# A schedule of eight-step slots for the attention groups, and other steps and layouts for the weight pieces, in a fused attention and two-layer MLP kernel

## Chip, cores and metric

One core of one Trainium2 chip runs the whole program. The metric is the device time of one execution in microseconds, the median of several.

## What is computed

Inputs: q, k, v of 8 batches x 8 heads x 576 tokens x 64, phi of 8 x 8 x 576 x 32, and four weight matrices.

```python
a = softmax(phi)                    # over the 32 memory slots of a token
k_m, v_m = a^T k, a^T v             # per head, 32 x 64
attn = softmax(q k_m^T / 8)         # 576 x 32
x = attn v_m                        # tokens x 512, 4608 tokens
h1 = x @ w1_in                      # 512 -> 2048
x1 = where(h1 > 0, h1, exp(min(h1, 0)) - 1) @ w1_out        # 2048 -> 512
h2 = x1 @ w2_in
out = (h2 * clip(h2 + 3, 0, 6) / 6) @ w2_out
```

Everything is float32.

## The kernel before

Every large product is made of three matmul passes over two fp32r parts of each operand (a "hi" part, which ScalarE casts, and a "lo" part, the rest): `three_passes`, lines 435 to 437, on PE. The program has four large passes, one after the other on PE: *up 1*, *down 1*, *up 2*, *down 2*. Between them the hidden values go to DRAM and come back.

**Up 1 with the attention (`batch`, 8 batches of 16 steps).** A step is one column block of the hidden layer: PE makes 12 matmuls of 128x288 (`up1`), ACT makes two activations (lines 771 and 773), DVE one operation (line 1053, `g_made`), SP stores the result (`store_h`). PE begins a step only when the g of two steps before is made. The product v_m x w1_in is not taken per token; it is folded into the weights: an *item* (8 per batch) is two plain matmuls on PE (line 524), a cast on ACT (763, hi part) and a difference on DVE (1044, lo part, `w1_lo_made`), and the next item waits for the lo part of the one before. The attention goes in groups of four heads, two groups per batch, 16 in all. Groups 0 and 1 are made in the *opening*, ahead of the first step. The others are made between the steps, cut into twelve stages: on the side of the values S_PHI (row maxima, DVE), S_MAX, S_SUB (DVE difference, ACT exponential), S_SUM (POOL), S_KV (24 matmuls, then two DVE operations for the inverse and copies on ACT and DVE), S_KMT (two transposes, copies of kmT and vT on ACT); on the side of the queries S_Q0, S_Q1 (six transposes each, copies on ACT and DVE), S_SC (24 matmuls, then two DVE operations), S_EXP (ACT), S_NORM (DVE, then `normalise` on POOL), S_PT (six transposes, then pT_hi on ACT and pT_lo on DVE).

What sets the order is a table written out by hand, `FIRST_BATCH` for batch 0 and `BATCH` for the others: at step f of batch b, `stages_at(b, f)` names the stages of the groups 2b+2 (EVEN), 2b+3 (ODD) and 2b+4 (NEXT); `items_at(b, f)` names the item. All five engines walk the same lists in the same order after their part of the step, each on its own instruction queue. In `BATCH`, S_SC stands at steps 4 and 10, S_PT at 9 and 15; items stand at steps 0, 2, 3 and, for the next batch, 5, 9, 11, 13 and 14. Step 0 of a batch waits for pT_lo of its own second group, which was made at step 15. The transposed scores and queries share two PSUM banks, so S_Q0 waits until pT_lo of the group before is made (EVEN) or other operations of it (ODD).

POOL also prepares *pieces* (`make_piece`): forms of w1_out and of a part of w2_out, seven sums of 128x128 blocks each in hi and lo, for a scheme with seven products in place of eight. SP loads the three blocks (`load_piece`), POOL makes sums, cast and difference, SP stores the piece to DRAM (`store_piece`). `PIECE_LOADS`, `PIECE_SUMS`, `PIECE_STORES` give their steps. Two pieces make a *tile* (1792 KB), eight tiles make a matrix. In DRAM a tile has 14336 contiguous bytes per partition, so `load_tile` moves 128 runs of 14336 bytes; a piece store moves runs of 7168 bytes.

**Down 1 (`y_block`, 9 blocks of 14 grains)** keeps the eight tiles of w1_out in SBUF; the pieces of w2_in go through `stage_b` meanwhile. In the last block ACT requests tiles 0 to 3 of w2_in one after the other (line 791, `load_tile(1, j)`), and tiles 4 to 7 after its casts for up 2. SP stores the last `y_sb` (layer 1's output), then waits for that store before it requests the input of batch 1 (`load_xc(1, 1)`) and goes on.

**Up 2 (`up_block`, 8 batches u of 8 steps f)**: a step is seven products of six matmuls 128x288. ACT copies one of them into `c_sum` (line 860, `up_first`), makes the gates (867) and the first activation into `eg` (876, `up_c11`); DVE makes the sums (1201 to 1226) and, at f == 2, the four sums of the next batch's input (`xc_sums`, 1184 to 1189); SP stores `eg` (`store_g`, line 1602). There are two `eg` buffers, and `up_c11` of step n waits until the store of step n-2 has landed. `c_sum` 1 and 2 and both `eg` share SBUF with `y_sb` or `stage_b`, so `up_first` of step 1 waits for the last store of `y_sb`. In batches 1 to 6 two pieces of w2_out are made per batch through the single `stage_c`: SP requests them ahead of steps 0 and 3 (`out_piece`, which first waits until the piece before it is stored), ACT casts at f == 2 and 7 (778), POOL makes sums and lo, SP stores at f == 2 and f == 7. SP's own queue is in order: `out_piece` at f == 0 stands ahead of `store_g(u, 0)`. In the last batch SP first requests three inputs of down 2 of 1 MB each (line 1627), then stores `eg`; ACT requests one tile of w2_out after each step (`load_tile(2, f - 1)`).

**Down 2 (`down_block`, 9 blocks of 14 grains)** uses these tiles; its second grain waits for tiles 4 to 7.

## Time and profile before

| what | us |
|---|---|
| median of 3 runs | 1719.53 |
| the runs | 1712.4 to 1724.2 |
| profiled execution, its time | 1714.28 |
| its span | 1712.6 |
| opening | 0 to 48 |
| up 1 with the attention | 48 to 518 |
| down 1 | 518 to 884 |
| up 2 | 884 to 1330 |
| down 2 | 1330 to 1712 |

The rows further down come from the profiled execution. Times in them count from the start of its span; 1.7 us of its time lie around the span. PE is TensorE (PEld its weight loads), DVE VectorE, ACT ScalarE, POOL GpSimd, SPq the queue of SyncE. "L437" is line 437. A bracket at the end of a timeline row is the engine's idle time before it and what ended it. PEclk is the granted TensorE clock as a share of 2.4 GHz.

### The profile page before, as it was taken

How to read it: one execution, taken by the hardware profiler on the slowest of the kernel's cores; microseconds unless marked ns; L12 is line 12 of the kernel's file. 1: busy time of each engine (PE TensorE's matmuls, PEld its weight loads, DVE VectorE, ACT ScalarE, POOL GpSimd, SP SyncE). 2: the span in 40 equal slices, each digit the busy share in tenths (PEclk: the TensorE clock that was granted, in tenths of full speed). 3: DMA queues.
4: the chain of work that ended last, by engine and by line, in shares of the span. 5: the costliest groups of instructions: out<-in, count | busy, mean ns of one | idle time of the engine just before them, and what ended most of it. 6: DMA issues, size and time to landing. Idle time of an engine off the chain costs nothing.

```text
span 1712.6 us, 30373 instructions
## 1 busy us (share of the span) xinstructions
PE 1537.7 (90%) x12080; PEld 1445.6 (84%) x12080; DVE 1098.6 (64%) x1528; ACT 730.2 (43%) x1037; POOL 262.1 (15%) x278
## 2 busy tenths in 40 slices
PE   6888887988979999999986999899987799999999
PEld 4666666766769999999986999899986799999998
DVE  4555555555547788888854666666645577777775
ACT  2555645555654444444422334343332333333333
POOL 0243433334200000000001233433220000000000
PEclk9989989998989999999997999999998899999999
DMA  8466678767576555555556444444468543333331
GB/s 243 145 189 213 208 244 263 222 229 231 198 265 239 194 184 178 197 189 178 172 228 250 150 162 170 147 154 179 160 223 313 192 135 129 122 122 122 122 126 46
DMA packets 193853, 318.26 MB, mean 186 GB/s; under 512 B 9456, under 2 KB 140528, under 8 KB 190704
## 3 DMA queue, kind: packets, MB, share of 16 engines
q1 hardware_dynamic: 189872, 285.81, 50.0%
q10 hardware_dynamic: 3904, 31.43, 5.0%
q8 instruction: 48, 0.79, 0.2%
q14 instruction: 29, 0.24, 0.0%
HBM read 178.78 MB, written 138.41 MB: 185 GB/s over the span
## 4 chain that ended last, share of the span: by engine, by line
PE 67%; DVE 11%; DMA 9%; ACT 6%; issue 4%; SPq 1%; POOL 0%; ACTq 0%; DVEq 0%
PE ps L435 21%; PE ps L437 20%; PE ps L436 20%; DMA layer_hidden<-eg 3%; PE ps L496 2%; DMA forms_out<-forms_c 2%; ACT e L773 2%; PE ps L524 2%; DVE g L1053 2%; ACT e L771 2%; PE ps L458 2%; DMA layer_out<-y_sb 1%; DVE ga_lo L1267 1%; DMA tile<-forms_out 1%; ACT ga_hi L918 1%
## 5 line engine op out<-in xcount | busy, mean ns | idle before, releaser
L435 PE MATMUL ps<-xc_hi,tile 128*128 128x288 f32 x896 | 275.0, 307 | 60.8 <-DVE c_sum L1201 58.5
L435 PE MATMUL ps<-tile,ga_lo 128*128 128x256 f32 x1008 | 288.9, 287 | 14.5 <-DMA tile<-forms_out 9.3
L435 PE MATMUL ps<-ring_hi,tile 128*128 128x256 f32 x1008 | 286.1, 284 | 3.0 <-DMA tile<-forms_out 3.0
L436 PE MATMUL ps<-tile,ga_hi 128*128 128x256 f32 x1008 | 287.0, 285 | 0.0
L437 PE MATMUL ps<-tile,ga_hi 128*128 128x256 f32 x1008 | 286.9, 285 | 0.0
L436 PE MATMUL ps<-ring_lo,tile 128*128 128x256 f32 x1008 | 285.2, 283 | 0.0
L437 PE MATMUL ps<-ring_hi,tile 128*128 128x256 f32 x1008 | 285.2, 283 | 0.0
L436 PE MATMUL ps<-xc_lo,tile 128*128 128x288 f32 x896 | 272.2, 304 | 0.0
L437 PE MATMUL ps<-xc_hi,tile 128*128 128x288 f32 x896 | 271.0, 302 | 0.0
L435 PEld LDWEIGHTS ps<-xc_hi,tile 128*128 128x128 f32 x896 | 175.8, 196 | 63.9 <-DVE c_sum L1201 61.1
L1053 DVE SCALAR_TENSOR_TENSOR g<-e,ps 128x576 f32<-128x576 f32 x128 | 95.7, 749 | 187.6 <-ACT e L773 180.0
L435 PEld LDWEIGHTS ps<-tile,ga_lo 128*128 128x128 f32 x1008 | 195.3, 194 | 17.9 <-issue 12.6
L435 PE MATMUL ps<-pT_hi,w_lo 128*128 128x288 f32 x512 | 168.0, 328 | 39.0 <-issue 18.9
L435 PEld LDWEIGHTS ps<-ring_hi,tile 128*128 128x128 f32 x1008 | 193.4, 192 | 3.5 <-issue 3.1
L436 PEld LDWEIGHTS ps<-tile,ga_hi 128*128 128x128 f32 x1008 | 195.4, 194 | 0.0
L437 PEld LDWEIGHTS ps<-tile,ga_hi 128*128 128x128 f32 x1008 | 195.2, 194 | 0.0
L436 PEld LDWEIGHTS ps<-ring_lo,tile 128*128 128x128 f32 x1008 | 193.5, 192 | 0.0
L437 PEld LDWEIGHTS ps<-ring_hi,tile 128*128 128x128 f32 x1008 | 193.5, 192 | 0.0
L437 PEld LDWEIGHTS ps<-xc_hi,tile 128*128 128x128 f32 x896 | 176.3, 197 | 0.0
L436 PEld LDWEIGHTS ps<-xc_lo,tile 128*128 128x128 f32 x896 | 176.1, 196 | 0.0
L918 ACT CAST ga_hi<-a 128x1024 fp32r<-128x1024 f32 x90 | 94.2, 1049 | 176.8 <-PE ps L437 154.6
L436 PE MATMUL ps<-pT_lo,w_hi 128*128 128x288 f32 x512 | 157.4, 307 | 0.0
(178 smaller groups left out, 2788.0 us busy)
## 6 DMA issues: line engine op xcount, KB each, us to landing
layer_hidden<-g SPq DMA_DIRECT2D x128, 288.0 KB, 2.7
x<-layer_hidden SPq DMA_DIRECT2D x36, 1024.0 KB, 5.1
layer_hidden<-eg SPq DMA_DIRECT2D x64, 576.0 KB, 3.0
a<-layer_hidden SPq DMA_DIRECT2D x36, 1024.0 KB, 7.4
forms_out<-forms_a SPq DMA_DIRECT2D x20, 896.0 KB, 4.5
tile<-forms_out SPq DMA_DIRECT2D x8, 1792.0 KB, 12.7
forms_in<-forms_b SPq DMA_DIRECT2D x16, 896.0 KB, 5.5
tile<-forms_in ACTq DMA_DIRECT2D x8, 1792.0 KB, 21.1
```

What stands on the lines that cost most here:

```text
L435: nc.tensor.matmul(dst, a_lo, b_hi, start=first, stop=False, skip_group_check=onto)
L436: nc.tensor.matmul(dst, a_hi, b_lo, start=False, stop=False, skip_group_check=onto)
L437: return nc.tensor.matmul(dst, a_hi, b_hi, start=False, stop=last, skip_group_check=onto)
L458: nc.tensor.matmul(t.ps_kv[rows], t.rows_a[0:ROWS, h, j], t.kv[0:ROWS, :, h, j], start=(j == 0), stop=(j == CH - 1))
L496: mm = nc.tensor.matmul(t.ps_scores[:, h, 2 * j:2 * j + 2], t.qT[:, h // 2, at:at + ROWS], t.kmT[:, h], start=True, stop=True)
L524: mm = nc.tensor.matmul(ps[lm, bank, 0:BANK], vT[:, gi, lm], w_in_raw[:, 2 * gi + p, cols], start=True, stop=True)
L771: nc.scalar.activation(e1[f % 2][:], ps[:, 2 * (f % 2):2 * (f % 2) + 2, 0:HALF], ACT.Relu, scale=-1.0).then_inc(r_made, 1)
L773: nc.scalar.activation(e1[f % 2][:], e1[f % 2][:], ACT.Exp, scale=-1.0).then_inc(e_made, 1)
L918: nc.scalar.copy(ga_hi[grain_slot(q)][:], grain_source(parity, q)).then_inc(grain_hi_made, 1)
L1053: nc.vector.scalar_tensor_tensor(g1[f % 4][:], e1[f % 2][:], -1.0, ps[:, 2 * (f % 2):2 * (f % 2) + 2, 0:HALF], ALU.add, ALU.max).then_inc( ...
L1267: nc.vector.tensor_tensor(ga_lo[slot][:], grain_source(parity, q), ga_hi[slot][:].bitcast(F32), ALU.subtract).then_inc(grain_ready, 1)
```

## The change

1. **Slots.** The two tables go. From batch 0, step 12 on, groups go in slots of eight steps that run on across batches: in the slot of group g its query stages stand at steps 0, 1, 2, 4, 5, 7 (Q0, Q1, SC, EXP, NORM, PT), and the value stages of group g+1 at 0, 1, 3, 4, 6, 7 (PHI, MAX, SUB, SUM, KV, KMT). With respect to a batch a slot begins at step 4 and at step 12. The first twelve steps of batch 0 are two slots of six. The value stages of group 2 are made in the opening (`EARLY`). Group 15 ends at step 11 of batch 6, before at 15.
2. **Items** at steps 1, 3 (the batch's own last two) and 5, 7, 9, 11, 13, 15 (six of the next batch) in plain order; in batch 0 at 0 to 3 and then the same. Six of a batch's items, not five, are made in the batch before. vT has four buffers, not two.
3. **Waits of PE.** S_Q0 always waits for pT_lo of the group before; the extra waits of S_SC and S_PT go.
4. **Pieces of w1_out**: loads at steps 0, 3, 9, sums at 2, 5, 11, stores at 4, 7, 14 (before 0, 6, 12; 2, 8, 14; 5, 11, 1).
5. **Layout** of the forms in DRAM: [j][s][l][partition][896], so each piece store and tile load moves runs of 3584 bytes (four per partition and tile).
6. **Start of up 2**: ACT requests tiles 0 and 1 in the last block of down 1, tile 2 after its casts, tiles 3 to 7 at steps 0 to 4. `y_sb` and `stage_b` trade places and `c_sum`, `eg` move, so that the last store of `y_sb` is waited for by `up_c11` of step 1 and `up_first` of step 2. SP requests `load_xc(1, 1)` ahead of its wait for that store.
7. **Batches 1 to 6 of up 2**: ACT's second cast and SP's second piece store go from f == 7 to f == 6. POOL's calls are written in another form in the same order.

```diff
-    forms = [nc.dram_tensor(f"forms_{n}", (FH, P, 2, 2 * 7 * P), F32, kind="Internal").ap() for n in ("out1", "in2", "out2")]
+    forms = [nc.dram_tensor(f"forms_{n}", (FH, 2, 2, P, 7 * P), F32, kind="Internal").ap() for n in ("out1", "in2", "out2")]
...
+        vT = place("vT", [4, P], F32, at + 2560)
...
-        at = t0 + 5 * TILE
+        at = tail - 2 * FB * WS - 2 * PT_BYTES
...
-        stage_b = stage("_b", tail + 3 * SUB * 8 + DC * BLOCK * 4)
+        stage_b = stage("_b", tail + 3 * SUB * 8)
...
-        y_sb = place("y_sb", [DC, BLOCK], F32, tail + 3 * SUB * 8)
+        y_sb = place("y_sb", [DC, BLOCK], F32, tail + 3 * SUB * 8 + PIECE)
...
-        c_sum = [place(f"c_sum{i}", [3, HALF], F32, tail + 3 * i * ring1) for i in range(3)]
-        eg = [place(f"eg{i}", [4, HALF], F32, tail + 3 * SUB * 8 + DC * BLOCK * 4 + 4 * i * ring1) for i in range(2)]
-        assert tail + 3 * SUB * 8 + DC * BLOCK * 4 + 8 * ring1 <= arena_bytes
+
+        c_sum = [place(f"c_sum{i}", [3, HALF], F32, tail + (0, 3, 10)[i] * ring1) for i in range(3)]
+        eg = [place(f"eg{i}", [4, HALF], F32, tail + (6, 13)[i] * ring1) for i in range(2)]
...
-        forms_rows = [f.rearrange("j p s x -> p j s x") for f in forms]
+        forms_rows = [f.rearrange("j s l p x -> p j s l x") for f in forms]
...
-        EVEN, ODD, NEXT = range(3)
-        FIRST_BATCH = {
-            0: ((S_MAX, EVEN),), 1: ((S_SUB, EVEN), (S_Q0, EVEN)), 2: ((S_SUM, EVEN), (S_Q1, EVEN)), 3: ((S_KV, EVEN),),
-            4: ((S_KMT, EVEN),), 5: ((S_SC, EVEN), (S_PHI, ODD)), 6: ((S_MAX, ODD),), 7: ((S_EXP, EVEN), (S_SUB, ODD)),
-            8: ((S_NORM, EVEN), (S_SUM, ODD), (S_Q0, ODD)), 9: ((S_KV, ODD), (S_Q1, ODD)), 10: ((S_PT, EVEN), (S_KMT, ODD)),
-            11: ((S_PHI, NEXT),), 12: ((S_SC, ODD), (S_MAX, NEXT)), 13: ((S_EXP, ODD), (S_SUB, NEXT)),
-            14: ((S_NORM, ODD), (S_SUM, NEXT)), 15: ((S_PT, ODD), (S_KV, NEXT))}
-        BATCH = {
-            0: ((S_KMT, EVEN),), 1: ((S_Q0, EVEN), (S_PHI, ODD)), 2: ((S_Q1, EVEN), (S_MAX, ODD)), 4: ((S_SC, EVEN),),
-            5: ((S_SUB, ODD),), 6: ((S_EXP, EVEN), (S_SUM, ODD), (S_Q0, ODD)), 7: ((S_NORM, EVEN),),
-            8: ((S_KV, ODD), (S_Q1, ODD)), 9: ((S_PT, EVEN), (S_KMT, ODD)), 10: ((S_SC, ODD), (S_PHI, NEXT)),
-            11: ((S_MAX, NEXT),), 12: ((S_EXP, ODD), (S_SUB, NEXT)), 13: ((S_SUM, NEXT), (S_NORM, ODD)),
-            14: ((S_KV, NEXT),), 15: ((S_PT, ODD),)}
+        EARLY = {S_SC: (S_PHI,), S_EXP: (S_MAX, S_SUB), S_NORM: (S_SUM,), S_PT: (S_KV, S_KMT)}
+
+
+
+        QUERIES = {0: (S_Q0,), 1: (S_Q1,), 2: (S_SC,), 4: (S_EXP,), 5: (S_NORM,), 7: (S_PT,)}
+        VALUES = {0: (S_PHI,), 1: (S_MAX,), 3: (S_SUB,), 4: (S_SUM,), 6: (S_KV,), 7: (S_KMT,)}
+        SHORT_QUERIES = {0: (S_Q0,), 1: (S_Q1,), 2: (S_SC,), 3: (S_EXP,), 4: (S_NORM,), 5: (S_PT,)}
+        SHORT_VALUES = {1: (S_PHI,), 2: (S_MAX,), 3: (S_SUB,), 4: (S_SUM,), 5: (S_KV,)}
         def stages_at(b, f):
-            found = (BATCH if b > 0 else FIRST_BATCH).get(f, ())
-            return [(stage, 2 * b + 2 + n, n) for stage, n in found if 2 * b + 2 + n < GROUPS]
-
-
-
-        NTH = (0, 2, 1, 4, 3, 6, 5, 7)
+            if b == 0 and f < 12:
+                group, s = 2 + f // 6, f % 6
+                queries, values = SHORT_QUERIES, SHORT_VALUES
+            else:
+                n = FC * b + f - 4
+                group, s = n // 8 + 3, n % 8
+                queries, values = QUERIES, VALUES
+            found = [(S_KMT, group)] if b == 0 and f in (6, 12) else []
+            found += [(stage, group) for stage in queries.get(s, ())] + [(stage, group + 1) for stage in values.get(s, ())]
+            return [(stage, g) for stage, g in found if g < GROUPS]
         def items_at(b, f):
...
-            ahead = {5: (1, 0), 9: (1, 1), 11: (1, 2), 13: (1, 3), 14: (1, 4)}
-            found = {0: (0, 5), 2: (0, 6), 3: (0, 7)} if b else {0: (0, 4), 1: (0, 5), 2: (0, 6), 3: (0, 7)}
-            found = {**ahead, **found}.get(f)
-            if found is None or b + found[0] >= B:
+
+            own = {1: 6, 3: 7} if b else {0: 4, 1: 5, 2: 6, 3: 7}
+            ahead = {5: 0, 7: 1, 9: 2, 11: 3, 13: 4, 15: 5}
+            if f in own:
+                n = own[f]
+            elif f in ahead and b + 1 < B:
+                b, n = b + 1, ahead[f]
+            else:
                 return []
-            n = found[1] if b + found[0] == 0 else NTH[found[1]]
-            return [(NI * (b + found[0]) + found[1], n, 2 * (b + found[0]) + n % 2)]
-
-
-        ITEMS_FOR = (3, 5, 7, 8)
-
-
-
-
-        PIECE_LOADS = {0: 0, 6: 1, 12: 2}
-        PIECE_SUMS = {2: 0, 8: 1, 14: 2}
-        PIECE_STORES = {5: 0, 11: 1}
+            return [(NI * b + n, n, 2 * b + n % 2)]
+
+
+
+        PIECE_LOADS = {0: 0, 3: 1, 9: 2}
+        PIECE_SUMS = {2: 0, 5: 1, 11: 2}
+        PIECE_STORES = {4: 0, 7: 1, 14: 2}
         PIECES = 2 * FH + 4
...
                         pe.wait_ge(q_copied_dve, nth(g, 0))
-                    elif not opening(g) and odd:
-
-                        pe.wait_ge(p_sub_step, 2 * g)
                     elif not opening(g):
+
                         pe.wait_ge(pT_lo_made, g)
...
-                    if not opening(g) and odd:
-
-                        pe.wait_ge(pT_lo_made, g)
...
-                    if not opening(g) and not odd:
-
-                        pe.wait_ge(q_copied_act, nth(g + 1, 1))
-                        pe.wait_ge(q_copied_dve, nth(g + 1, 1))
...
-                    pe.wait_ge(w1_lo_made, PRE if t == 0 else NI * b + ITEMS_FOR[f // FS])
+                    pe.wait_ge(w1_lo_made, PRE if t == 0 else NI * b + 2 * (f // FS + 1))
...
+                for early in EARLY.get(stage, ()):
+                    attention(2, early, A)
...
-                            for j in range(FH // 2):
+                            for j in range(2):
                                 load_tile(1, j)
...
-                elif isinstance(n, int) and n == 1:
+                elif isinstance(n, int) and n == 2:
                     act.wait_ge(stored, 16 * BLOCKS)
...
-                if isinstance(n, int) and n < 2:
+                if isinstance(n, int) and n == 0:
                     act.wait_ge(stage_b.stored, 16 * 2 * FH)
+                elif isinstance(n, int) and n == 1:
+                    act.wait_ge(stored, 16 * BLOCKS)
...
+                    if first and f + 3 < FH:
+                        if f == 1:
+                            act.wait_ge(xg_used, GRAINS * BLOCKS)
+                        load_tile(1, f + 3)
...
-                    if not first and not last and f in (2, 7):
-                        piece_hi(stage_c, 2 * (u - 1) + f // 7)
+                    if not first and not last and f in (2, 6):
+                        piece_hi(stage_c, 2 * (u - 1) + f // 6)
...
-            for j in range(FH // 2, FH):
-                act.wait_ge(xg_used, GRAINS * BLOCKS)
-                load_tile(1, j)
+            load_tile(1, 2)
...
-            attention(2, S_PHI, A, 2)
...
+            row_sums(2, A)
...
-                sp.dma_start(dst[:, bass.ds(j, 1), s], st.both[:].rearrange("p (o l) f x -> p o (l f x)", o=1)).then_inc(st.stored, 16)
+                sp.dma_start(dst[:, bass.ds(j, 1), s].rearrange("p o l x -> p (o l) x"), st.both[:].rearrange("p l f x -> p l (f x)"))\
+                    .then_inc(st.stored, 16)
...
-                sp.dma_start(tile[j][:].rearrange("p s l f x -> p s (l f x)"), forms_rows[n][:, j]).then_inc(tile_loaded[j], 16)
+                sp.dma_start(tile[j][:].rearrange("p s l f x -> p (s l) (f x)"), forms_rows[n][:, j].rearrange("p s l x -> p (s l) x"))\
+                    .then_inc(tile_loaded[j], 16)
...
-                    if f == 1 and piece(b - 1, 2) is not None:
-                        store_a(piece(b - 1, 2))
...
-                    if makes and f == 7:
+                    if makes and f == 6:
...
+            follow_kv(2, 3)
...
+            load_xc(1, 1)
             sp.wait_ge(stored, 16 * BLOCKS)
-            load_xc(1, 1)
```

(In the same way `odd` and the third member of the lists of `stages_at` go, on every engine; ACT's `load_tile` changes as SP's does.)

## Rows read from the trace of the kernel before

**Rows 1.** the page, busy time, share and instructions of each engine

```profile
PE 1537.7 (90%) x12080; PEld 1445.6 (84%) x12080; DVE 1098.6 (64%) x1528; ACT 730.2 (43%) x1037; POOL 262.1 (15%) x278
```

**Rows 2.** windows: length; busy us (and count) PE, PEld, DVE, ACT, POOL; PEclk; DMA share; GB/s

```profile
242.00:300.00 58.00, 48.90 (x420) 39.40 (x416) 33.25 (x60) 34.16 (x62) 20.37 (x25) 0.97 0.77 243
...
1268.00:1342.00 74.00, 45.47 (x299) 44.35 (x299) 36.23 (x58) 16.69 (x25) 0.00 (x0) 0.84 0.91 319
```

**Rows 3.** timeline of ACT, first activation of eight steps: start, length, [idle before, releaser]

```profile
51.62 0.65 ACT L771 ACTIVATE e<-ps 128x576 f32<-128x576 f32 x1 [4.60 <-PE ps L437]
...
120.38 0.65 ACT L771 ACTIVATE e<-ps 128x576 f32<-128x576 f32 x1 [1.56 <-PE ps L437]
...
245.12 0.65 ACT L771 ACTIVATE e<-ps 128x576 f32<-128x576 f32 x1 [0.69 <-PE ps L437]
...
250.88 0.65 ACT L771 ACTIVATE e<-ps 128x576 f32<-128x576 f32 x1 [1.51 <-PE ps L437]
...
253.69 0.65 ACT L771 ACTIVATE e<-ps 128x576 f32<-128x576 f32 x1 [0.96 <-PE ps L437]
...
273.60 0.66 ACT L771 ACTIVATE e<-ps 128x576 f32<-128x576 f32 x1
...
421.82 0.65 ACT L771 ACTIVATE e<-ps 128x576 f32<-128x576 f32 x1 [3.87 <-PE ps L437]
...
475.65 0.65 ACT L771 ACTIVATE e<-ps 128x576 f32<-128x576 f32 x1 [3.52 <-PE ps L437]
```

**Rows 4.** timeline of PE, end of the fourth batch

```profile
288.62 1.08 PE L524 MATMUL ps<-w_in_raw,vT 128*64 128x512 f32 x4 [2.31 <-DVE w_lo L1044]
...
297.02 0.37 PE L435 MATMUL ps<-pT_hi,w_lo 128*128 128x288 f32 x1 [3.36 <-issue]
```

**Rows 5.** timeline of PE, the opening

```profile
24.04 0.59 PE L461 MATMUL ps<-stats,rows_sum_b 96*128 96x1 f32 x2
...
26.05 0.45 PE L465 MATMUL ps<-ident,kvm_b 128*128 128x128 f32 x1 [0.90 <-ACT kvm_b L741]
```

**Rows 6.** timeline of ACT, first activation into eg of seven steps of layer 2

```profile
889.72 0.50 ACT L876 ACTIVATE eg<-ps,stats 128x288 f32<-128x288 f32 x1 [2.56 <-PE ps L437]
...
936.41 0.50 ACT L876 ACTIVATE eg<-ps,stats 128x288 f32<-128x288 f32 x1
...
942.01 0.50 ACT L876 ACTIVATE eg<-ps,stats 128x288 f32<-128x288 f32 x1
...
970.01 0.50 ACT L876 ACTIVATE eg<-ps,stats 128x288 f32<-128x288 f32 x1
...
979.92 0.50 ACT L876 ACTIVATE eg<-ps,stats 128x288 f32<-128x288 f32 x1 [1.59 <-PE ps L437]
...
1072.10 0.50 ACT L876 ACTIVATE eg<-ps,stats 128x288 f32<-128x288 f32 x1 [2.89 <-DMA layer_hidden<-eg]
...
1122.49 0.50 ACT L876 ACTIVATE eg<-ps,stats 128x288 f32<-128x288 f32 x1 [1.49 <-DMA layer_hidden<-eg]
```

**Rows 7.** the chain that ended last, layer 2: start, length, what

```profile
886.77 23.05 DMA layer_out<-y_sb
...
1060.11 7.04 DMA forms_out<-forms_c
...
1270.19 5.63 SPq L1627
...
1275.92 10.19 DMA layer_hidden<-eg
...
1330.97 8.55 DMA tile<-forms_out
```

**Rows 8.** DMA queues in 890 to 900 us: packets, MB, share

```profile
q10 hardware_dynamic: 285, 3.63, 85.2%
q1 hardware_dynamic: 274, 0.56, 14.5%
```

**Rows 9.** the page, DMA issues: count, KB each, median us to landing

```profile
x<-layer_hidden SPq DMA_DIRECT2D x36, 1024.0 KB, 5.1
```

More of the change, by code:

```diff
@@ L748, in attention @@
                     op.then_inc(kmT_copied, 1)
-                    nc.scalar.copy(vT[:, slot % 2], t.ps_vT).then_inc(vT_made, 1)
+                    nc.scalar.copy(vT[:, slot], t.ps_vT).then_inc(vT_made, 1)
                 elif stage in (S_Q0, S_Q1):
@@ L946, in _ @@
                 attention(1, stage, B_, 1)
+                for early in EARLY.get(stage, ()):
+                    attention(2, early, A, 2)
                 if stage in (S_SC, S_NORM):
@@ L1324, in _ @@
                 attention(1, stage, B_, 1)
+                for early in EARLY.get(stage, ()):
+                    attention(2, early, A, 2)
                 if stage in (S_SC, S_NORM):
@@ L1408, in batch @@
                 for f in range(FC):
-                    for stage, g, n in stages_at(b, f):
+                    for stage, g in stages_at(b, f):
                         if stage == S_SUM:
@@ L1426, in up_block @@
                 makes = not isinstance(u, int) or u > 0
-                for n in range(4):
-                    if makes and n in (0, 2):
-                        right_sums(stage_c, 2 * (u - 1) + n // 2)
-                    if makes and n == 0:
-                        piece_lo(stage_c, 2 * (u - 1))
+                if makes:
+                    right_sums(stage_c, 2 * (u - 1))
+                    piece_lo(stage_c, 2 * (u - 1))
+                for n in range(2):
+                    xc_split_lo(u + 1, 1 - buf, n)
+                if makes:
+                    right_sums(stage_c, 2 * (u - 1) + 1)
+                for n in range(2, 4):
                     xc_split_lo(u + 1, 1 - buf, n)
@@ L1514, in batch @@
                     store_h(b, f)
-                    for stage, g, n in stages_at(b, f):
+                    for stage, g in stages_at(b, f):
                         if stage == S_KV and g + 1 < GROUPS:
```

24 lines of the change are left out of this document (13 added, 11 removed).

## Prediction

> **What bounds the kernel now.** I read the page first: TensorE is busy for 90% of the span [rows 1], so at most 10% can be won without taking work from it, and the change takes none from it. The slices of the page show where the rest is: down 1 and down 2 run full, up 1 and two short places around up 2 don't. I then read windows of those places. In the fourth batch of up 1 PE is busy for 48.9 of 58 us, at a granted clock of 0.97 of 2.4 GHz [rows 2], so there PE waits for the other engines, whose chains are long, not full (ACT 34 of 58 us, DVE 33). In 1268 to 1342 us, the end of up 2, PE is busy for 45 of 74 us while the DMA engines are at 0.91 [rows 2]: that stretch is bound by transfers. The timeline of PE and the chain that ended last say what ends each wait.
>
> **Up 1: slots and items.** A batch is read from the start of ACT's first activation. Batches 1 to 5 take (421.82 - 120.38) / 5 = 60.3 us, batch 0 68.8, batch 6 53.8 [rows 3]. In the old table the end of a batch is the costly part: an item follows an item by one step and waits 2.31 us for w1_lo, and step 0 waits 3.36 us for pT_lo made at step 15 [rows 4]. Items at every second step end the first wait, and S_PT now stands at steps 3 and 11, so nothing at a batch's edge waits for it.
>
> What is late next I take from steps of the old batch that hold the same stages as a slot's. Old steps 1 and 2 (Q0 with PHI; item, Q1, MAX) are slot steps 0 and 1: 245.12 to 250.88, 5.8 us. Old steps 4 to 9 (SC; item, SUB; EXP, SUM, also Q0; NORM; KV, also Q1; item, PT, KMT) are slot steps 2 to 7: 253.69 to 273.60, 19.9 us [rows 3]. Together 25.7 us. Three corrections. The slot has one more item (step 5, 1.08 us [rows 4]) and lacks the second Q0 and the second Q1, which I put at about an item's length each. The Q0 lay beside the long ACT work of its step (SUB's exponential, then EXP), so only the Q1 comes off: with the item 0 (bounds -1.1 and +1.1). The fourth batch is shorter than the mean (58.6 us, nearly the window of rows 2, for 60.3): half of that, 0.9, is added. And Q0 now comes one step after S_PT and waits for its pT_lo, before two steps after: the bounds are 0 and the 3.36 us of the old wait for the same operation; PE makes the 12 matmuls of a step in between (1.6 us, as the 42 of a step of up 2 take 5.6 [rows 6]), and ACT's kmT and vT copies stand behind pT_hi, not ahead, so I take 1.0. A slot is 27.6 us, a batch 55.2: 5.1 us less, in five batches **-25.5** (bounds: no wait and a full PE 49 us, so -11 a batch; the 3.36 us wait in each slot 60, so 0).
>
> Batch 6 keeps half of group 14 (half a slot, 13.8 us less the values) and the queries of 15 (a slot without values, 22.6 by taking KV, SUB and their waits at 5 us); its last four steps are bare or hold an item only, 1.6 and 2.7 us, 8.6. That is some 44 us for 53.8; I take **-8** (-5 to -11), as part of the work has only moved to earlier batches. Batch 7 loses an item, **-1**; its long wait is a store behind loads on SP, which stays.
>
> Batch 0 gets the queries Q0, Q1, SC of group 4, three stages of group 5 and one more item, and loses the values of group 2: by the count of operations some 3 us more of PE. Its slots of six leave EXP, NORM (DVE, then POOL) and PT on three neighbouring steps, a wait that I put between the 2.31 and 3.36 us of rows 4 in each; against that the waits of the old batch's edge go. I take **-1.5** (-6 to +4).
>
> The opening gets the values of group 2. DVE gets PHI, MAX and SUB ahead of the first NORM, which I put at 1.5 us beyond its idle time, PE goes through KV and then waits for its copies, as in the old opening from the sum at 24.04 to the transpose at 26.05, 2.0 us [rows 5]; pT_lo of group 1 hides the KV itself. **+3.5** (+1 to +5). The later SP and POOL calls of a slot (phi and k, v for the next group behind S_KV, two steps ahead of PHI; q a slot ahead; pieces at 2, 5, 11, between SUM and NORM) leave each landing more than one step of slack, and SP's wait for a piece at step 4 is covered by the four g1 buffers: 0, up to 1 us a batch if not.
>
> Up 1 and opening: -25.5 - 8 - 1 - 1.5 + 3.5 = **-32.5 us**.
>
> **Start of up 2.** A step of up 2 is 5.6 us (936.41 to 942.01); step 0's activation at 889.72 would put step 4's at 912.1, and it is at 936.41 [rows 6]: 24.3 us lost. The chain shows why: the last y_sb store takes 23.05 us [rows 7], all eight tile loads being ahead. In 890 to 900 us ACT's queue moved 285 packets of 12.7 KB on average, SP's 274 of 2.0 KB [rows 8]: the DMA engines alternate packet by packet, whatever the size. The store has 512 rows of 2048 B, 32 per engine, and 4.19 MB in 10 us is 26 KB/us per engine: 32 x (14.3 + 2.05) / 26 = 20 us, plus 2 to 3 us around it. That fits. With runs of 3584 B it is 32 x (3.6 + 2.05) / 26 = 7 us, 9.5 in all: it lands near 896, and `up_c11` of step 1, due at 895.3, hardly waits. But load_xc(1, 1) is now ahead of the first eg store in the same queue: 64 runs of 1152 B per engine beside tiles, 64 x (1.15 + 3.6) / 26 = 11.7 us, then 16 runs of 2304 B, 3.6 us. So the eg store of step 0 lands near 911, and step 2, due at 900.9, waits 10 us. From there two more steps and the sums give 924 for step 4: -12; I take **-11** (-3 to -18).
>
> By the Trainium skill (DMA: Bandwidth & Descriptors, "Queues, rings and completion order") an engine drains a whole packet of about 9 to 17 descriptors of one ring before it switches. Rows 8 don't show that, with one for one; by that rule a shorter run would change little, and only the later requests would help.
>
> **Middle of up 2.** SP's out_piece at f == 0 waits for the store of the piece before (7.04 us [rows 7]), with the eg store of step 0 behind it, and ACT at f == 2 idles 2.89 us for that store [rows 6]. With the piece store one step (5.6 us) earlier it has landed by then, and the eg store goes out on time. Batch 1, which has no piece before it, shows what is left: 9.91 us from f == 2 to f == 3 [rows 6], because the four sums stand in DVE's queue beside POOL's. A period of 50.39 us [rows 6] becomes 44.8 + 4.4 = 49.2. The ACT cast at f == 6 comes 0.9 us before the next c_sum copy, which PE wants two products later: 0. Five periods by 1.2 to 2.1 us, near 1.4: **-7** (0 to -10).
>
> **End of up 2.** The three 1 MB requests held SP for 5.63 us and the first eg store behind them took 10.19 us [rows 7]. The earlier piece store lets SP request them about 5 us, nearly a step, earlier. But the stretch moves 0.91 of what DMA can [rows 2], so shorter eg waits are mostly given back: what moves is the start. The last tile (8.55 us [rows 7]) is unchanged. **-5** (-1 to -14).
>
> Down 1 and down 2 run full on PE, and their transfers lie beside it: 0.
>
> **Sum.** -32.5 - 11 - 7 - 5 = -55.5 us on the profiled execution's 1714.3 gives 1658.8. That execution stands 5.2 us under the median of the runs; from the median 1719.5 it is **1664 us**.
>
> **Rivals.** (a) Slots give back what they take: Q0 waits the full 3.36 us for pT_lo twice a batch. For it: S_PT's two long operations are on ACT and DVE, in line with g; against it: a whole step lies between. Then a batch is 60, up 1 gives only the batch 6 part, and the time is 1664 + 26 = 1690.
> (b) Run length does not matter to the arbitration. Against it: rows 8. Start of up 2 gives 5, not 11, its end 2: 1673. The skill's rule above would bring this.
> (c) Slower: four times as many descriptors make a tile load slow. Alone it takes 8.55 us [rows 7], 6.5 without 2 us around it; at half the rate 15. Then the eight loads at the start of up 2 pace it, 13 us each: from 877 on the last lands near 981, where step 7 before was at 953 (942.01 and two steps [rows 6]): 28 us later. The end of up 2 has seven loads of 6.5 us more, 45, and the last tile of down 1 6.5. That is +79.5 against -39.5 from up 1 and the middle, 1760. It decides from half of this, a lone load of 11.8 us. Against it: 1 MB in runs of 1024 B lands in 5.1 us [rows 9]. By the skill (the same page, "Why small descriptors are slow (HBM only)") the cost of a packet is 3 cycles beside its 32-byte beats, 112 of them for 3584 B: an estimate of 2%.
> (d) PE hardly waits in the slots: 52 us a batch, 1648.
>
> **Chances.** Forecast 0.50, (a) 0.20, (b) 0.12, (c) 0.07, (d) 0.11. Of (a), the part with longer waits, 0.07, falls within 1% of before (1702 to 1737, about what a measurement tells from no change). Faster 0.86, same 0.07, slower 0.07. The range 1638 to 1698 leaves out (c), the tail of (a) and the best of (d).
>
> **What would show it.** Up 1: ACT's first activations some 55 us apart per batch, even over the two slots, the first step at 52 us, not 48; PE idle before Q0's transposes about 1 us (right) or over 3 (a). Start of up 2: the y_sb store near 9 us and the largest wait at the activation of step 2, about 10 us. Middle: no wait for layer_hidden at f == 2, but the 9.9 us step still there. End: the first eg store of the last batch still near 10 us. A lone tile load over 11 us would be (c). The forecast is wrong if batches stay at 60 us, or if up 2 starts no earlier.

## The result, and the profile after

The changed kernel takes 1655.99 us (median of 4 runs, 1652.44 to 1665.84) beside 1721.87 for the kernel before on the same chip: a ratio of 0.9632 over all the runs, 95% interval 0.9568 to 0.9695 (the two medians alone give 0.9617). The forecast was 1664, with a range of 1638 to 1698. The profiled execution took 1659.14 us (span 1657.4), 55.1 less than the 1714.28 of before; the forecast's sum was -55.5. That near match holds for these two executions: the one of before stands 7.6 us under its median, the one of after 3.2 above. Over all runs the ratio is worth 63 us, 53 to 74 by its interval.

The page, engines: busy time, share and instructions. PE does the same 12080 matmuls as in [rows 1], but its busy time is 16.1 us less, at a mean granted clock of 0.970 for 0.957. So part of the 55.2 us of span is a faster PE and not a shorter wait.

```profile
PE 1521.6 (92%) x12080; PEld 1433.1 (86%) x12080; DVE 1102.4 (67%) x1528; ACT 729.4 (44%) x1037; POOL 264.9 (16%) x278
```

Windows, one batch of up 1 and the end of up 2, with the columns of [rows 2]. In up 1 PE is now busy for 48.0 of 55 us (48.9 of 58 before); the end of up 2 is still a stretch of transfers, at 0.94.

```profile
295.00:350.00 55.00, 47.95 (x421) 38.41 (x420) 33.92 (x61) 34.52 (x63) 21.18 (x26) 1.00 0.84 260
1214.00:1266.00 52.00, 42.80 (x295) 42.16 (x294) 29.28 (x54) 13.11 (x22) 0.00 (x0) 0.90 0.94 329
```

The same for batches 1 to 5 of up 1 together, before and after. Of the 27.2 us that they lose, 13.7 are busy time of PE for the same matmuls, with the clock up from 0.94 to 0.99, and 13.4 are idle time.

```profile
120.38:421.82 301.44, 254.44 (x2092) 204.03 (x2092) 168.99 (x300) 173.09 (x311) 106.04 (x130) 0.94 0.75 235
126.82:401.10 274.28, 240.72 (x2093) 193.04 (x2092) 171.93 (x300) 172.02 (x312) 106.50 (x130) 0.99 0.82 254
```

Timeline of ACT, the first activation of batches 0 to 3, 6 and 7, as in [rows 3]:

```profile
55.88 0.65 ACT L764 ACTIVATE e<-ps 128x576 f32<-128x576 f32 x1 [2.04 <-PE ps L437]
...
126.82 0.63 ACT L764 ACTIVATE e<-ps 128x576 f32<-128x576 f32 x1
...
179.81 0.63 ACT L764 ACTIVATE e<-ps 128x576 f32<-128x576 f32 x1
...
236.57 0.63 ACT L764 ACTIVATE e<-ps 128x576 f32<-128x576 f32 x1
...
401.10 0.63 ACT L764 ACTIVATE e<-ps 128x576 f32<-128x576 f32 x1
...
444.96 0.65 ACT L764 ACTIVATE e<-ps 128x576 f32<-128x576 f32 x1 [0.96 <-PE ps L437]
```

Batch 1 takes 52.99 us. Batch 2 takes 56.76, and batches 2 to 5 all have one longer step, step 13 counted from 0: 6.88, 5.63, 5.55 and 5.09 us, for 3.35 in batch 1. The timeline of batch 2 (start, length, engine; the bracket as before) shows what happens there:

```profile
217.37 1.18 DVE L1039 TENSOR_TENSOR pT_lo<-ps,pT_hi 128x576 fp32r<-128x576 f32 x1 [0.26 <-ACT pT_hi L752]
...
218.59 0.71 PE L479 MATMUL ps<-ident,q 96*128 96x96 f32 x6 [1.27 <-DVE pT_lo L1039]
...
221.69 0.75 DVE L987 TENSOR_TENSOR fold<-rows_a 96x384 f32<-96x384 f32 x1 [1.22 <-DMA rows_a<-in_phi]
...
222.10 2.26 POOL L1395 TENSOR_TENSOR forms_a<-forms_a 128x896 fp32r<-128x896 f32 x1
...
222.47 2.04 DVE L989 TENSOR_TENSOR row_max<-fold 96x128 f32<-96x128 f32 x1
```

DVE's PHI waits for phi, whose request at 213.51 stands behind a tile load of 1792 KB on SP's queue, put there at step 8. Being late, PHI falls beside POOL's long operation, and 96x128 elements take 2.04 us. PE then stands 2.31 us for the row maxima, and its matmuls behind that wait (225.4 to 228.0 us) run at a granted clock of 0.51. The wait of Q0 for pT_lo, which I had put at 1.0 us, is 1.27.

Batch 0 takes 70.94 us for 68.76, with two steps of 11.1 and 11.6 us at the end of the short slots. Batch 0 of before has two such steps too, 10.2 us at step 9 and 11.4 at step 15. Timeline of POOL and PE there:

```profile
76.56 1.48 POOL L1367 TENSOR_TENSOR rows_p<-rows_p,stats 96x768 f32<-96x768 f32 x1 [10.67 <-DVE stats L1036]
78.00 1.00 POOL L1359 TENSOR_TENSOR fold<-rows_a 96x384 f32<-96x384 f32 x1
...
78.09 0.72 PE L497 MATMUL ps<-ident,rows_p 96*128 96x96 f32 x6 [3.74 <-POOL rows_p L1367]
```

PE waits 3.74 us at PT for `normalise`, and POOL makes the SUM that the next KV needs only after it. PE does not wait for that SUM, though: it is made at 80.05, and PE comes to it at 81.47, straight from KV's other matmuls. What follows the wait is a low clock. The window behind it (columns of [rows 2]):

```profile
78.09:86.00 7.91, 7.91 (x77) 7.23 (x78) 2.39 (x6) 2.80 (x6) 6.58 (x9) 0.57 0.57 171
```

In the second short slot the wait is 4.18 us, and the clock in 103 to 111 us is 0.50.

Layer 2: the chain that ended last (start, length, what), as in [rows 7]:

```profile
856.76 12.88 DMA layer_out<-y_sb
...
869.65 15.82 DMA layer_hidden<-eg
...
1021.28 7.45 DMA layer_hidden<-eg
...
1221.27 12.90 DMA layer_hidden<-eg
...
1239.53 8.56 DMA layer_hidden<-eg
```

Timeline of ACT, the first activation into eg of steps 0 to 4, then three steps of batch 2 and three of batch 3, as in [rows 6]:

```profile
859.80 0.50 ACT L872 ACTIVATE eg<-ps,stats 128x288 f32<-128x288 f32 x1 [2.64 <-PE ps L437]
...
869.72 0.50 ACT L872 ACTIVATE eg<-ps,stats 128x288 f32<-128x288 f32 x1 [3.96 <-DMA layer_out<-y_sb]
...
885.56 0.50 ACT L872 ACTIVATE eg<-ps,stats 128x288 f32<-128x288 f32 x1 [12.44 <-DMA layer_hidden<-eg]
...
893.17 0.50 ACT L872 ACTIVATE eg<-ps,stats 128x288 f32<-128x288 f32 x1 [1.59 <-PE ps L437]
...
899.41 0.50 ACT L872 ACTIVATE eg<-ps,stats 128x288 f32<-128x288 f32 x1
...
980.81 0.50 ACT L872 ACTIVATE eg<-ps,stats 128x288 f32<-128x288 f32 x1 [0.20 <-PE ps L437]
...
990.64 0.50 ACT L872 ACTIVATE eg<-ps,stats 128x288 f32<-128x288 f32 x1 [1.59 <-PE ps L437]
...
997.62 0.50 ACT L872 ACTIVATE eg<-ps,stats 128x288 f32<-128x288 f32 x1 [0.20 <-PE ps L437]
...
1028.81 0.50 ACT L872 ACTIVATE eg<-ps,stats 128x288 f32<-128x288 f32 x1 [3.39 <-DMA layer_hidden<-eg]
...
1032.19 0.50 ACT L872 ACTIVATE eg<-ps,stats 128x288 f32<-128x288 f32 x1 [0.28 <-PE ps L437]
...
1040.62 0.50 ACT L872 ACTIVATE eg<-ps,stats 128x288 f32<-128x288 f32 x1 [0.20 <-PE ps L437]
```

At the start of up 2, steps 0 to 4 take 39.6 us for 46.7. In the middle the wait for the eg store has moved from f == 2 to f == 1 (3.39 us at 1028.81), and the step after it is short by as much. From f == 2 to f == 3 batch 3 takes 8.43 us, batch 2 9.83 and then 6.98. Windows of those two places (columns of [rows 2]) show the difference: a granted clock of 0.68 on average in one, full speed, 2.4 GHz, in the other.

```profile
987.00:997.00 10.00, 9.65 (x52) 9.65 (x53) 4.99 (x11) 3.39 (x5) 2.66 (x1) 0.68 0.39 152
1038.00:1048.00 10.00, 9.27 (x69) 9.27 (x70) 7.26 (x15) 5.22 (x7) 2.69 (x1) 1.00 0.40 152
```

| stretch, profiled executions | before | after | difference | forecast |
|---|---|---|---|---|
| opening, to the first activation | 51.62 | 55.88 | +4.3 | +3.5 |
| batch 0 | 68.76 | 70.94 | +2.2 | -1.5 |
| batches 1 to 5 | 301.44 | 274.28 | -27.2 | -25.5 |
| batch 6 | 53.83 | 43.86 | -10.0 | -8 |
| batch 7 | 40.71 | 39.56 | -1.2 | -1 |
| from there to up 2's first activation | 373.36 | 375.28 | +1.9 | 0 |
| up 2, batch 0 | 69.10 | 62.01 | -7.1 | -11 |
| up 2, batches 1 to 6 | 303.7 | 292.7 | -11.0 | -7 |
| up 2, last batch, first to last activation | 58.85 | 52.16 | -6.7 | -5 |
| from there to the end | 391.20 | 390.76 | -0.4 | 0 |

### The profile page after: what moved, and what is told of

Same layout as the page of the kernel before. It is cut to its first block, busy times and chain, and to the rows that moved or that the text cites. A ratio compares the mean times of both kernels' runs of the same rounds, so it can differ in the third digit from the quotient of the medians.

```text
span 1657.4 us, 30358 instructions
## 1 busy us (share of the span) xinstructions
PE 1521.6 (92%) x12080; PEld 1433.1 (86%) x12080; DVE 1102.4 (67%) x1528; ACT 729.4 (44%) x1037; POOL 264.9 (16%) x278
## 4 chain that ended last, share of the span: by engine, by line
PE 69%; DVE 12%; DMA 8%; ACT 7%; issue 3%; POOL 0%; SPq 0%; ACTq 0%; DVEq 0%
PE ps L435 22%; PE ps L437 21%; PE ps L436 21%; DMA layer_hidden<-eg 3%; PE ps L491 2%; ACT e L764 2%; DMA rows_a<-in_phi 2%; DVE g L1053 2%; ACT e L766 2%; DVE ga_lo L1267 1%; DVE w_lo L1044 1%; DMA kv<-in_v 1%; PE ps L515 1%; ACT ga_hi L918 1%; PE ps L458 1%
## 5 line engine op out<-in xcount | busy, mean ns | idle before, releaser
L435 PE MATMUL ps<-xc_hi,tile 128*128 128x288 f32 x896 | 271.9, 303 | 41.6 <-DVE c_sum L1201 37.9
L437 PE MATMUL ps<-xc_hi,tile 128*128 128x288 f32 x896 | 268.3, 299 | 0.0
L435 PEld LDWEIGHTS ps<-xc_hi,tile 128*128 128x128 f32 x896 | 172.8, 193 | 45.0 <-DVE c_sum L1201 40.4
L435 PE MATMUL ps<-pT_hi,w_lo 128*128 128x288 f32 x512 | 164.2, 321 | 21.7 <-DVE g L1053 21.7
L437 PEld LDWEIGHTS ps<-xc_hi,tile 128*128 128x128 f32 x896 | 173.3, 193 | 0.0
## 6 DMA issues: line engine op xcount, KB each, us to landing
tile<-forms_in ACTq DMA_DIRECT2D x8, 1792.0 KB, 13.7
```

What stands on the lines that cost most here:

```text
L435: nc.tensor.matmul(dst, a_lo, b_hi, start=first, stop=False, skip_group_check=onto)
L437: return nc.tensor.matmul(dst, a_hi, b_hi, start=False, stop=last, skip_group_check=onto)
```

## The experiments

The theory after the first reading: the two halves of the change, slots and layer 2, act apart and add; in up 1 the slots win what they should, less what late phi loads and the short slots cost; in layer 2 the two load queues and the stores share the DMA engines packet by packet, so that shorter runs let a store through. Rivals: the halves share one gain; the layout does nothing and the later requests all. Ten kernels were run. Not all ran on one chip, so I compare whole times as ratios to the kernel before on the same chip, and single stretches in the profiles.

**Each half alone.** The first has parts 1 to 4 (slots, items, waits, pieces of w1_out), the second parts 5 to 7. The first, in short:

```diff
+        QUERIES = {0: (S_Q0,), 1: (S_Q1,), 2: (S_SC,), 4: (S_EXP,), 5: (S_NORM,), 7: (S_PT,)}
...
```

The second:

```diff
+    forms = [nc.dram_tensor(f"forms_{n}", (FH, 2, 2, P, 7 * P), F32, kind="Internal").ap() for n in ("out1", "in2", "out2")]
...
+                        load_tile(1, f + 3)
...
```

> The changed kernel with layer 2 and the DRAM layout as before (only parts 1 to 4: slots, items, PE's waits, pieces of w1_out). Theory A (each part acts in its own stretch): up 1 is as in the changed kernel (batches 1 to 5 about 54.9 us each, opening to 56 us) and the rest as before, so 32 us less than before, near 1690 for 1722. Rival B (the gains lean on each other: with runs of 14336 B the tile loads of up 1 hold up the loads of phi, k, v and q, which the slots want two steps after their request): batches 2 to 5 go back towards 58 us and no more than 20 us is left.

> The kernel before with only parts 5 to 7 (layout, start of up 2, middle of up 2), the old tables. Theory A: the start of up 2 gives 7 us, the middle 11, the end 7, together 24 less than before, near 1698. Rival B (the shorter up 1 only shifted transfers that now fit better around up 2): less than 15.

Slots only: 1686.6 us, ratio 0.9825 (0.9787 to 0.9864); layer 2 only: 1684.52, ratio 0.9816 (0.9779 to 0.9853). The product is 0.9644, the whole change has 0.9632: the halves add. With slots only the y_sb store still takes 23.23 us and batches 1 to 5 take 53.0 to 58.0, together 3.8 more than in the change; with layer 2 only they take 58.7 to 61.7, the y_sb store 12.72 and the eg store behind it 15.84. Slots only gives 30 us by its ratio, near the 32 expected. Layer 2 only gives 32 where 24 were expected. Its profile says where: the start of up 2 gives 7.5 us and the end 5.7, but batches 1 to 6 take 286.99 us, 16.7 less than before and not 11. In the kernel before each of these six batches has a spell of lower clock (0.85 or 0.92 over f == 1 to 4), with layer 2 only none has.

**The layout, from both sides.** First the changed kernel with the old layout:

```diff
-    forms = [nc.dram_tensor(f"forms_{n}", (FH, 2, 2, P, 7 * P), F32, kind="Internal").ap() for n in ("out1", "in2", "out2")]
+    forms = [nc.dram_tensor(f"forms_{n}", (FH, P, 2, 2 * 7 * P), F32, kind="Internal").ap() for n in ("out1", "in2", "out2")]
...
```

> The changed kernel with the old DRAM layout alone (tile loads in runs of 14336 B, piece stores in 7168 B). Theory A (the DMA engines alternate one packet of each queue, whatever its size): the last y_sb store of layer 1 takes until the tiles ahead of it are through, about 16 us or more, the first eg store later still, and the eg stores of the last batch of up 2 between tile loads 9 us; the whole is 8 us slower than the changed kernel (4 to 15). Rival B (run length does not matter, only the later requests and the earlier piece store help): within 2 us of the changed kernel, and the same two stores take 13 and 16 us as there.

1667.23 us, ratio 0.9698 (0.9651 to 0.9745), 0.0066 or 11 us above the change, with intervals that overlap a little. Its chain at the start of up 2:

```profile
860.92 19.99 DMA layer_out<-y_sb
...
886.25 10.28 DMA layer_hidden<-eg
```

The y_sb store is slower, as theory A has it, but what stands behind it is faster. SP requests the store of eg 0 at 880.93 us, and step 2's activation at 885.56 no longer waits for it, only 1.46 us for PE; the 10.28 us are the store of eg 1, for which step 3 waits 5.02 us. From the request of the y_sb store to the activation of step 4 it is 41.4 us, in the change 42.7; batch 0 of up 2 takes 60.45 us for 62.01. So at the start of up 2 the layout wins nothing, and the whole gain there comes from part 6: with neither (slots only) this batch takes 67.54. In the profiles the kernel is 9.2 us longer than the change, and that lies elsewhere: the last batch of up 2 +3.6 (eg stores 12.59, 10.63 and 9.48 us), batches 2 and 3 of up 1 +3.1 (the step with PHI takes 7.8 and 7.6 us), the middle of up 2 +2.8 (where spells of a lower clock play in, below), the opening +1.1.

Then the layout alone, in the kernel before:

```diff
-    forms = [nc.dram_tensor(f"forms_{n}", (FH, P, 2, 2 * 7 * P), F32, kind="Internal").ap() for n in ("out1", "in2", "out2")]
+    forms = [nc.dram_tensor(f"forms_{n}", (FH, 2, 2, P, 7 * P), F32, kind="Internal").ap() for n in ("out1", "in2", "out2")]
...
```

> The kernel before with part 5 alone: the layout of layer 2's inputs in memory, nothing else. Theory A (the two load queues and a store share the DMA engines one packet for one, so the size of the other queue's packets sets how long a small store takes): at the start of up 2 the y_sb store falls from 23 to 10 to 13 us, the last batch's eg stores from 9.4 to 10.2 to about 8.5, the whole is 5 to 18 us faster than before. Rival B (what counts at the start of up 2 is the bytes queued, whatever their packets): within 3 us of before, since what the y_sb store gains the next store gives back; the earlier pair of runs (the change with the old layout lost 11 us, of which little at the start of up 2) speaks for a part at other places only.

1713.17 us (12 runs), ratio 0.9991 (0.9972 to 1.0011): rival B's number. Yet not by rival B's mechanism. Timeline of ACT and of SP's queue at the start of up 2:

```profile
888.60 7.49 ACTq L791 DMA_DIRECT2D tile<-forms_in  x1
...
896.13 10.87 ACTq L791 DMA_DIRECT2D tile<-forms_in  x2
907.11 0.40 ACT L861 COPY c_sum<-ps 128x288 f32<-128x288 f32 x1 [16.99 <-issue]
...
893.34 0.39 SPq L1566 DMA_DIRECT2D layer_out<-y_sb  x1
904.66 0.37 SPq L1597 DMA_DIRECT2D xc_raw<-layer_out  x1
```

SP's next request, which waits for the y_sb store, goes out 11.3 us after the store's, where the store took 23.05 [rows 7]: the size of the other queue's packets does set a small store's time (524 packets of SP's queue to 534 of ACT's in 897 to 904 us). But the last three tile requests now hold ACT itself for 18.4 us, so that its first copy for up 2 waits 16.99 us. In the kernel before the last three together took 1.5 us. From the first tile request to step 4's activation it is 57.9 us (882.43 to 940.36) for 59.3 before (877.10 to 936.41). Eight tiles are 1152 packets in the old layout and 4224 in the new one in these windows; that ACT waits for room in its queue is my reading, the rows show only how long the requests take. In the changed kernel, where tiles 3 to 7 are requested one by one after steps, each takes 0.4 to 0.5 us. So with all the requests in a row the gain of the y_sb store is not passed on. What the layout is worth beside part 6 is not settled: the 11 us above have overlapping intervals, and here the last batch of up 2 gains 2.1 us while the middle, with a low-clock spell in all six batches as before, is 2.8 longer.

**The phi wait of batches 2 to 5.** The tile load of these batches goes from step 8 to step 12, behind the request for phi.

```diff
-                if 2 <= b < 6 and f == 8:
+                if 2 <= b < 6 and f == 12:
```

> The changed kernel with the tile loads of batches 2 to 5 (SP, 1792 KB) at step 12 and not at step 8, so behind the requests for phi, k and v at step 10. Theory A (the steps after step 13 of batches 2 to 5, 5.1 to 6.9 us, wait for phi, which stands behind the tile in SP's queue; batch 1, without a tile load, takes 53.0 us, they take 54.7 to 56.8): these batches fall to about 53 us, 8 to 9 us less in all than the changed kernel. Rival B (the DMA engines are the limit in these batches and the wait only moves): 0 to 2 us.

1645.64 us, ratio 0.9597 (0.9554 to 0.9640). The interval overlaps that of the change, but the place is plain: batches 1 to 5 take 53.02, 53.04, 53.05, 53.06 and 53.29 us, 8.8 less together. DVE, in the same place of batch 2:

```profile
220.95 0.55 DVE L987 TENSOR_TENSOR fold<-rows_a 96x384 f32<-96x384 f32 x1
221.53 0.29 DVE L989 TENSOR_TENSOR row_max<-fold 96x128 f32<-96x128 f32 x1
```

No wait for phi, and the operation of 2.04 us takes 0.29 clear of POOL's. The two profiles differ by more, 15.5 us: 5.7 of it are in the middle of up 2, where this edit changes nothing but no batch meets the lower clock (286.99 us for 292.67).

**Batch 0's short slots.** In steps 4 and 5 of both short slots, the value stages stand ahead of the query stages, so POOL makes SUM before NORM and PE does KV before PT.

```diff
-            found += [(stage, group) for stage in queries.get(s, ())] + [(stage, group + 1) for stage in values.get(s, ())]
+            own = [(stage, group) for stage in queries.get(s, ())]
+            ahead = [(stage, group + 1) for stage in values.get(s, ())]
+            found += ahead + own if b == 0 and f < 12 and s in (4, 5) else own + ahead
```

> The changed kernel; in batch 0's short slots, steps 4 and 5 list the value stages ahead of the query stages. Theory (PE's wait of 3.74 us at PT for POOL's normalise, and POOL's SUM behind it, make these steps 11 us long): batch 0 falls from 70.9 to 64 to 66 us, the whole by 5 to 7 us. Rival (the wait is only replaced, by KV's for its copies or the first step's loads): batch 0 stays at 70 to 72, the whole within 2 us.

1646.05 us, ratio 0.9591 (0.9565 to 0.9618), 0.0041 or 7 us under the change, within its wide interval; the profile decides. Batch 0 takes 63.11 us for 70.94: its two steps of 11.1 and 11.6 us are 8.2 and 6.4. What is left of the wait, timeline of PE:

```profile
76.76 1.22 PE L499 MATMUL ps<-ident,rows_p 96*128 96x96 f32 x6 [2.36 <-POOL rows_p L1369]
```

In the second slot it is 2.42. KV's 48 matmuls now run ahead of the wait and at full speed, 1.52 us for 2.79. The clock is 0.50 behind the first wait (76.76 to 82.00 us), but 1.00 behind the second (100 to 108), where it was 0.50. The size is the theory's, and a little more (63.11 for 64 to 66); its reason is in part another, since PE had not waited for POOL's SUM.

**The order of the requests at the start of up 2.** The store of eg 0 goes ahead of `load_xc(1, 1)`. (That load is 1152 KB of input; the expectation calls it a weight load of 2.4 MB.) As the eg store stands behind SP's wait for the y_sb store, the load now goes out 13 us after the y_sb request, at 868.80 us, and not 0.4 us after it.

```diff
-            load_xc(1, 1)
...
-            up_block(0, 0, makes=False)
+            up_block(0, 0, makes=False, then={0: lambda: load_xc(1, 1)})
```

> The changed kernel; at the start of up 2 the first hidden-layer store is issued ahead of the weight load of the next chunk, not behind it. Theory (the store takes 15.8 us since it is queued behind that load's 2.4 MB and a tile): the store takes 5 to 8 us, the first interval of 39.6 us for four steps falls by 3 to 8 us, the whole by as much. Rival (the start of up 2 is bound by the bytes that must arrive, so that the sums of inputs at the third step wait as much later): the whole within 2 us of the changed kernel.

1662.23 us, ratio 0.9669 (0.9640 to 0.9699): above the change by 6 us, which the overlapping intervals leave unclear; in any case none of the theory's gain. The activation of step 2, which waits for the eg store, comes 8.33 us after that of step 1, not 15.84, and that of step 3 then 18.48 us later, not 7.61. The chain says why:

```profile
870.09 18.37 DMA xc_raw<-layer_out
```

The sums at f == 2 wait for the input instead, and longer. Batch 0 of up 2 takes 65.52 us for 62.01. The DMA engines have a share of 1.03 or more from 855 to 885 us, so up to there the bytes that must arrive bind the stretch, and the order chooses who waits; the change had the better one. Behind the long wait PE's clock is 0.50 (885 to 895 us), which adds to the loss.

**Batch 7's wait.** The kernel with the tiles at step 12, and the first inputs of down 1 three steps earlier, at step 14 of batch 6.

```diff
-                elif (b, f) == (7, 1):
+                elif (b, f) == (6, 14):
```

> The changed kernel with the tile loads of up 1 at step 12 (as in the earlier run of 1645.6 us) and the first inputs of down 1 requested one step earlier. Theory (the last batch of up 1 waits 6.7 to 7.7 us for a store that is queued behind these inputs): that wait falls below 4 us and the whole is 3 to 5 us below 1645.6. Rival (the inputs only come to lie beside another store or piece): within 2 us of 1645.6, the wait stays above 6.

1644.68 us, ratio 0.9592 (0.9568 to 0.9616), against 0.9597: no difference, and the rival is right. The long step of batch 7 is 10.08 us at step 4 instead of 7.68 at step 7; the store that it waits for takes 10.75 us for 11.49.

**Two edits together.** Tiles at step 12 and the values first in the short slots; and that kernel with the two quadrants for down 2 requested behind the first and the second store of the last batch of up 2, not ahead of both.

```diff
-            load_quad(a22, 0, 1, 1, a22_loaded)
-            load_quad(a11, 0, 0, 0, a11_loaded)
-            up_block(B - 1, 1, makes=False, follows=False)
+            up_block(B - 1, 1, makes=False, follows=False,
+                     then={0: lambda: load_quad(a22, 0, 1, 1, a22_loaded), 1: lambda: load_quad(a11, 0, 0, 0, a11_loaded)})
```

> The changed kernel with two edits at once: the tile loads of up 1's batches 2 to 5 at step 12, and the value stages ahead of the query stages in batch 0's two short slots. Theory (the two act on different batches of up 1 and add): batches 2 to 5 at 53.0 us each, batch 0 at 63 to 64, the whole at 1637 to 1640 us. Rival (they draw on the same slack): no better than either alone, 1645 to 1647.

> The kernel of the run before it, and in the last batch of up 2 the two quadrants for down 2 are requested behind the first and second hidden-layer store instead of ahead of both. Theory (the stretch is bound by the bytes that down 2 needs, and down 2's own wait for its inputs takes what the stores give): the first of the three store waits falls from some 12 to 5 to 8 us and the whole gains at most 3 us. Rival (the stores alone set the end): 6 to 10 us faster than the run before it.

The first: 1638.97 us, ratio 0.9547 (0.9523 to 0.9571), 0.0050 under the tiles alone and 0.0044 under the short slots alone, some 8 us each: they add. Batch 0 takes 63.96 us, batches 2 to 5 53.02 to 53.30. The second: 1635.15 us, ratio 0.9532 (0.9508 to 0.9556), 3.8 us less on the same chip, with intervals that overlap. Its chain at the end of up 2:

```profile
1197.31 7.63 DMA layer_hidden<-eg
...
1209.55 13.19 DMA layer_hidden<-eg
...
1230.34 8.37 DMA layer_hidden<-eg
```

The first of these stores is 7.63 us for the 12.90 of the change, the one for step 2 13.19 for 8.56, and the last batch takes 51.61 us for the 52.06 of the first kernel. That is the theory of a stretch bound by bytes, and the rival's 6 to 10 us are out. So the 3.8 us are not shown to be the edit's: of the 9.3 us between the two profiles 7.4 are in the middle of up 2, where the first kernel has four low-clock spells and the second none. Both beat the change, by 0.0085 and 0.0100 of the time of before, 15 and 17 us; the interval of the second ends below that of the change, that of the first just touches it.

## Why the prediction came out

The two halves and their places are as forecast. The close total is in part luck: terms miss by up to 4 us both ways, and the executions profiled happened to lie 55 us apart where all runs give 63. One step of the forecast fails through all its terms: "at most 10% can be won without taking work from it" took PE's busy time as fixed, and it fell by 16.1 us with no work taken, by a higher granted clock.

**Slots (-25.5, measured -27.2).** The order of the stages acts as forecast, but half of the gain is clock (above), for which the sum has no term of its own. Undisturbed, a batch is 53.0 us, not 55.2, as batch 1 and all five batches of the kernel with tiles at step 12 show. The sum of the old steps and the wait, 25.7 + 1.0 us, is right for a slot of 26.5; too dear was the 0.9 added because the fourth batch is shorter than the mean. The step that failed is "leave each landing more than one step of slack": phi is late behind the tile load of 1792 KB in SP's queue, which costs 8.8 us over batches 2 to 5. The ten times 0.9 us nearly cancel it, and that is luck. Rival (d), 52 us a batch, was the nearer for the slots by themselves; (a) is out, Q0 waits 1.27 us, at most 1.6.

**Batch 0 (-1.5, measured +2.2).** I put a wait "between the 2.31 and 3.36 us of rows 4" in each short slot. It is 3.74 and 4.18 us, and behind it PE runs at a clock of 0.57 and 0.50, so that KV's matmuls, all behind the wait, take 2.79 us for 1.52. Reordering gave 7.8 us back. I had priced the wait, somewhat low, and neither the clock after it nor the work that could have run under it.

**Batch 6, 7 and the opening (-5.5, measured -6.9)**: as forecast, within 2 us each (-10.0 for -8, -1.2 for -1, +4.3 for +3.5).

**Start of up 2 (-11, measured -7.1).** The places were right: the larger wait, 12.44 us, is at the activation of step 2 (forecast 10), and the eg store takes 15.82. The y_sb store took 12.88 us, not 9.5. The failed term is the "2 to 3 us around it". Counts of the two queues (packets, MB, share) in four windows, 857 to 860, where ACT's is alone, 860 to 861, 862 to 869 and 869 to 877:

```profile
q10 hardware_dynamic: 358, 1.23, 103.4%
...
q10 hardware_dynamic: 94, 0.34, 86.0%
q1 hardware_dynamic: 30, 0.06, 15.9%
...
q10 hardware_dynamic: 545, 1.90, 66.8%
q1 hardware_dynamic: 542, 0.98, 36.4%
...
q10 hardware_dynamic: 702, 2.46, 76.1%
q1 hardware_dynamic: 702, 0.77, 27.3%
```

The store is requested at 856.76 and its first packets stand in 860.25 to 860.5: some 3.6 us. (In the kernel before it is as long, from 886.77 to 890.25 to 890.5.) Its 512 packets at 542 in 7 us then take 6.6, the 7 us that I had, so 6.3 us lie around them. The store is 3.4 us longer than forecast, steps 0 to 4 together 5.3. The counts are one for one, at 3.5 KB against 1.8 and against 1.1 KB, so the share by count, whatever the size, that the forecast used holds. By the Trainium skill (DMA: Bandwidth & Descriptors, "Queues, rings and completion order") about 9 to 17 descriptors of a ring go in one packet before the engine switches; these counts, like [rows 8], don't show that. They don't show the contrary either, as I took them to: turns of equal groups give equal counts as turns of one do. So my step from that rule to "a shorter run would change little" does not follow. What failed beside the size is the credit: rival (b), "Run length does not matter", had 5 us at this place. Run length does matter to the store (19.99 us with the old layout, 12.88 with the new), yet the layout won nothing here: what the y_sb store wins, the eg stores behind it lose. Part 6 gave it all.

**Middle (-7, measured -11).** The piece store no longer holds the eg store at f == 2, as forecast; a wait of about 3 us appears at f == 1 instead, and the next step takes it back. The mis-sized term is "batch 1, which has no piece before it, shows what is left: 9.91 us". That step held a spell at a lower granted clock (mean 0.83 in 970 to 980 us of before; 1.00 in 936 to 946 after, the same place of batch 1, where the step takes 8.52). Without a spell the batch is 47.7 us, with one 50.4. The change met one in 2 of its 6 batches, the kernel before in all 6 (0.85 or 0.92 over f == 1 to 4), so part of the -11 is clock, not wait: PE's busy time falls by 5.9 us. Without any spell the middle gives 16.7 us. No run has part 7 alone, so its share in that is not shown.

**End (-5, measured -6.7).** The first eg store takes 12.90 us, longer than forecast ("near 10"), the later one on the chain 8.56 for 9.5, and the chain no longer ends on a tile. With the old layout the batch takes 55.80 us for 52.16, and the layout alone takes 2.1 us off the old one, so 2 to 4 us of the gain are the layout's. The share of DMA time is still 0.94, and spreading the quadrants won little in this batch (0.4 us): bound by bytes.

**Rival (c)**, slow tile loads by shorter runs, is out: the last tile of down 1 lands after 8.91 us, where it took 8.38 before; it would have had to be over 11.

## What to carry to other kernels

When a stage moves, follow the loads that feed it through the queue they stand in: a load of 1.8 MB requested ahead of a small one cost 8.8 us here over four batches. In a stretch that is bound by bytes, order and packet size mostly choose which transfer waits and not how long the stretch is, so read the sum of the waits on the chain, not the one that got shorter. A layout with more and shorter runs lets a small store through (23.05 us to 11.3), but eight such requests at once held the engine that issued them, and the whole gained nothing. And compare PE's busy time and granted clock by stage before a gain is put down to shorter waits: half of the gain of the slots was clock.
